# Attention with its last 64 keys as one product per pair of heads, and the first pair's prologue moved into the step lists

## What is computed

```python
# attention: B, H, S, D = 2, 8, 576, 64
scores = scale * np.matmul(q, k.transpose(0, 1, 3, 2))      # causal
a = exp(scores - max); a /= a.sum(-1) + 1e-9
local = np.matmul(a, v)
q_p = phi(q)                                                # max(q, 0) + min(exp(q), 1)
mem_out = (q_p @ M_prev) / (q_p . z_prev + 1e-6)
g = sigmoid(beta)
out = g * mem_out + (1 - g) * local
# then x = out as 1152 x 512: softplus(x @ w_in) @ w_out, and a mixture of 8 experts
```

## Time and profile before

| | |
|---|---|
| median of 3 runs | 1118.59 us (1118.3 to 1119.08) |
| the profiled execution | 1118.5 us, span 1116.5 us |
| granted TensorE clock, mean | 0.998 |
| PE busy | 1104.0 us (99%) |
| DVE, ACT, POOL busy | 703.5, 489.7, 434.4 us |
| attention (first to last pair's products) | up to about 147 us of the span |

### The profile page before, as it was taken

The page is one execution under the profiler, slowest core; times in us unless marked ns, Lnnn a source line. Parts: engine busy times, 40 slices in busy tenths (PEclk is TensorE's granted clock), DMA queues, the critical chain, the costliest instruction groups (busy, mean ns, idle before and its releaser), DMA issues.

```text
span 1116.5 us, 20453 instructions
## 1 busy us (share of the span) xinstructions
PE 1104.0 (99%) x6722; PEld 1004.2 (90%) x6722; DVE 703.5 (63%) x1319; ACT 489.7 (44%) x1061; POOL 434.4 (39%) x487
## 2 busy tenths in 40 slices
PE   7999999999999999999999999999999999999998
PEld 5889899999997989999899999999899899898997
DVE  5988743353377787666656666565675756657564
ACT  5888865575465333533333323333233332333331
POOL 5898800001044244253433534344352442524421
PEclk9999999999999999999999999999999999999999
DMA  4334122002001110101112011110111101111001
GB/s 110 90 98 108 32 76 75 1 1 77 0 20 38 38 47 30 57 23 54 57 38 56 19 56 56 38 56 19 56 56 38 56 19 56 53 39 41 19 10 76
DMA packets 65933, 52.78 MB, mean 47 GB/s; under 512 B 32480, under 2 KB 53984, under 8 KB 65888
## 3 DMA queue, kind: packets, MB, share of 16 engines
q1 hardware_dynamic: 65456, 52.13, 15.6%
q10 hardware_dynamic: 432, 0.07, 0.0%
HBM read 49.83 MB, written 2.36 MB: 47 GB/s over the span
## 4 chain that ended last, share of the span: by engine, by line
PE 94%; DVE 2%; issue 1%; POOL 1%; DMA 0%; ACT 0%; SPq 0%; ACTq 0%; POOLq 0%; DVEq 0%
PE ps_y L1474 40%; PE ps_h L1474 27%; PE ps_g L1474 17%; PE ps_o L1474 4%; PE ps_p L1512 2%; PE ps_s L1488 2%; PE ps_s L1474 0%; PE ps_y L1706 0%; DMA k_nat<-in_k_dram 0%; DVE zl L1235 0%; PE ps_t L1455 0%; PE ps_t L1459 0%; DVE acc L1355 0%; PE ps_g L1706 0%; PE ps_t L1466 0%
## 5 line engine op out<-in xcount | busy, mean ns | idle before, releaser
L898 ACT ACTIVATE zh<-h 128x256 fp32r<-128x256 f32 (+1 forms) x256 | 112.3, 444 | 329.3 <-POOL h L674 134.1
L1474 PE MATMUL ps_y<-w2c_h,zh 128*128 128x512 f32 x512 | 202.7, 396 | 0.0
L1474 PE MATMUL ps_y<-w2c_l,zh 128*128 128x512 f32 x512 | 201.8, 394 | 0.0
L1474 PE MATMUL ps_y<-w2c_h,zl 128*128 128x512 f32 x512 | 199.3, 389 | 0.0
L669 POOL TENSOR_TENSOR h<-u,p 128x256 f32<-128x256 f32 (+1 forms) x64 | 57.0, 891 | 361.9 <-DVE u L1212 361.9
L1235 DVE SCALAR_TENSOR_TENSOR zl<-h,zh 128x256 fp32r<-128x256 f32 (+1 forms) x256 | 173.1, 681 | 8.7 <-ACT zh L898 8.4
L1474 PEld LDWEIGHTS ps_y<-w2c_h,zl 128*128 128x128 f32 x512 | 96.2, 188 | 21.9
L1474 PEld LDWEIGHTS ps_y<-w2c_h,zh 128*128 128x128 f32 x512 | 96.6, 189 | 13.4
L1474 PEld LDWEIGHTS ps_y<-w2c_l,zh 128*128 128x128 f32 x512 | 96.6, 189 | 11.8
L1363 DVE SCALAR_TENSOR_TENSOR acc<-ps_y,weight,acc 128x512 f32<-128x512 f32 x112 | 82.2, 743 | 37.2 <-PE ps_y L1474 37.2
L674 POOL TENSOR_TENSOR h<-h,p 128x256 f32<-128x256 f32 (+1 forms) x64 | 60.9, 952 | 101.7 <-DVE h L1223 101.7
(11 more groups left out here) (243 smaller groups left out, 3056.2 us busy)
## 6 DMA issues: line engine op xcount, KB each, us to landing
rc<-in_moe_w_dram SPq DMA_DIRECT2D x64, 512.0 KB, 3.7
out_dram<-acc SPq DMA_DIRECT2D x9, 256.0 KB, 2.0
q_nat<-in_q_dram SPq DMA_DIRECT2D x16, 128.0 KB, 2.6
k_nat<-in_k_dram SPq DMA_DIRECT2D x16, 128.0 KB, 2.8
v_nat<-in_v_dram SPq DMA_DIRECT2D x16, 128.0 KB, 2.4
raw<-in_moe_w_in_dram SPq DMA_DIRECT2D x8, 256.0 KB, 3.0
raw<-in_moe_w_out_dram SPq DMA_DIRECT2D x8, 256.0 KB, 3.0
raw<-in_moe_w_in_dram SPq DMA_DIRECT2D x1, 2048.0 KB, 7.8
```

The costliest lines, as they stand in the source:

```text
L898: act.activation(z_place(u, quarter, 0), rows, ACT.Relu).then_inc(e_hi, 1)
L1474: last = pe.matmul(dst, a[x], b[y], start=start and i == 0, stop=stop and i == 2)
```

## The change

1. **One product for both heads' last keys.** The last 64 rows of v no longer go to `v_nat` (which keeps 4 blocks) but by one DMA per head into a second half of `mem_nat`, at the diagonal block of the head. `mem_h` and `mem_l` have two halves as well, split by the same two instructions, now of 256 columns; `vh` and `vl` shrink from 5 to 4 blocks. The transposed probabilities of the second head's tail go to partitions 64 to 127, which takes two instructions in place of one in `probs_hi` and `probs_lo` for the last part. `values(4, 1)` is then one product of full height: three matmuls of 256 columns in place of six of half height.
2. **The prologue as steps.** The straight code ahead of the lists is gone; its pieces stand in the first lists as `first`, `gate`, `relu0`, `phi0`, `keep0`, `split0`, `early`, in another order: GpSimd has `split0` 0 (`vh`, `mem_h`) ahead of `times_z`, `split0` 1 (`mem_l`) right after it, and `split0` 2 (`vl`) after `norm` 1; ScalarE has `relu` and `phi` ahead of `first` 2; VectorE has the norms ahead of `max` 2 and the row sums. The number of matmuls on zeros stays 22.
3. **Loads of the first pair.** q and k for both heads first (`ld_q0`, `ld_k0`), then both tails (`ld_t0`), then `z_prev` on SyncE's queue; `prep` 0 and 1 wait for the heads alone.
4. **New orders** in all eight lists. `split_v` has three parts, `keep` is a step of its own. In `PE_STEPS` "pt" 3 stands right behind "pt" 2, and "memory" 0 ahead of "prep" 3.

```diff
 PE_STEPS = [
-    ("qk", 5), ("pt", 2), ("qk", 6), ("pt", 3), ("prep", 3), ("memory", 0), ("pt", 4), ("pt", 5),
-    ("values", (0, 0)), ("values", (0, 1)), ("prep", 4), ("pt", 6), ("pt", 7),
+    ("qk", 5), ("pt", 2), ("pt", 3), ("qk", 6), ("memory", 0), ("prep", 3), ("pt", 4), ("pt", 5), ("values", (0, 0)),
+    ("values", (0, 1)), ("prep", 4), ("pt", 6), ("pt", 7),
 ]
 PE_FIRST = [
-    ("qk", 2), ("awake", 0), ("qk", 3), ("awake", 1), ("awake", 2), ("first", 3), ("awake", 3), ("qk", 4),
-    ("first", 4), ("prep", 0), ("pt", 0), ("pt", 1), ("prep", 1), ("awake", 4), ("awake", 5), ("memory", 0),
-    ("pt", 2), ("prep", 2), ("qk", 5), ("pt", 3), ("qk", 6), ("pt", 4), ("pt", 5), ("prep", 3), ("values", (0, 0)),
-    ("pt", 6), ("values", (0, 1)), ("prep", 4), ("pt", 7),
+    ("early", 0), ("early", 1), ("early", 2), ("early", 3), ("first", 0), ("first", 1), ("first", 2), ("qk", 0),
+    ("qk", 1), ("awake", 0), ("awake", 1), ("awake", 2), ("qk", 2), ("awake", 3), ("qk", 3), ("awake", 4),
+    ("first", 3), ("awake", 5), ("qk", 4), ("pt", 0), ("first", 4), ("prep", 0), ("pt", 1), ("pt", 2), ("memory", 0),
+    ("prep", 1), ("values", (0, 0)), ("pt", 3), ("prep", 2), ("pt", 4), ("qk", 5), ("qk", 6), ("values", (0, 1)),
+    ("prep", 3), ("pt", 5), ("pt", 6), ("prep", 4), ("pt", 7),
 ]
 DVE_STEPS = [
-    ("phi", 3), ("sum", 3), ("parts", 0), ("parts", 1), ("item", 2), ("sum", 4), ("x", -1), ("parts", 2),
+    ("parts", 0), ("phi", 3), ("parts", 1), ("sum", 3), ("x", -1), ("item", 2), ("max", 5), ("keep", 0), ("parts", 2),
...
 POOL_FIRST = [
+    ("split0", 0), ("phi0", 2), ("split0", 1), ("eps", 0), ("eps", 1), ("phi0", 4), ("norm", 0), ("norm", 1),
+    ("split0", 2), ("eps", 2), ("norm", 2), ("norm", 3), ("norm", 4), ("norm", 5), ("eps", 3), ("phi", 2),
+    ("norm", 6), ("split", 0), ("eps", 4), ("phi", 4), ("norm", 7), ("norm", 8), ("split", 1), ("eps", 5),
+    ("split", 2), ("weights", 0), ("norm", 9),
 ]
...
-            return to[1][0:TAIL, :, 4, 2 * P:2 * P + QB], bank[0:TAIL, 0:P].rearrange("p (h c) -> p h c", h=2)
+            rows = slice(h * QB, (h + 1) * QB)
+            return to[1][rows, 0, 4, 2 * P:2 * P + QB], bank[0:TAIL, rows]
...
+                if dst is v_nat:
+                    for h in range(2):
+                        sp.dma_start(mem_nat[h * QB:(h + 1) * QB, 1, h * D:(h + 1) * D],
+                                     both[h:h + 1, NT * P:S, :].rearrange("o p d -> p (o d)")).then_inc(done, 16)
+            def load_first():
+                for dst, src, done in ((q_nat, q3, ld_q0), (k_nat, k3, ld_k0)):
+                    for h in range(2):
+                        sp.dma_start(dst[:, 0:NT, h * D:(h + 1) * D],
+                                     src[h:h + 1, 0:NT * P, :].rearrange("o (j p) d -> p (o j) d", p=P))\
+                            .then_inc(done, 16)
+                for dst, src in ((q_nat, q3), (k_nat, k3)):
+                    sp.dma_start(dst[0:TAIL, NT, :].rearrange("p (h d) -> p h d", h=2),
+                                 src[0:2, NT * P:S, :].rearrange("h p d -> p h d")).then_inc(ld_t0, 16)
+                sp.dma_start(z_nat[:, 0, :], z3[:, 0:P].broadcast_to([P, P])).then_inc(ld_z[0], 16)
...
-                rows = slice(0, P if j < NT else TAIL)
-                for h in range(2):
-                    v_of = [x[rows, half, j, h:h + 2, :].rearrange("p a d -> p (a d)") for x in (vh, vl)]
-                    last = products(ps_o[:, c:n], v_of, [x[g][rows, h, j, c:n] for x in (pth, ptl)],
-                                    False, j == GKEYS[g] - 1 and h == 1)
+                if j < NT:
+                    for h in range(2):
+                        v_of = [x[:, half, j, h:h + 2, :].rearrange("p a d -> p (a d)") for x in (vh, vl)]
+                        last = products(ps_o[:, c:n], v_of, [x[g][:, h, j, c:n] for x in (pth, ptl)],
+                                        False, j == GKEYS[g] - 1 and h == 1)
+                else:
+                    last = products(ps_o[:, c:n], (mem_h[:, half, 1, :], mem_l[:, half, 1, :]),
+                                    [x[g][:, 0, j, c:n] for x in (pth, ptl)], False, True)
```

More of the change, by code:

```diff
@@ L37 @@
 ]
 ACT_FIRST = [
[L39 to L42, removed]
+    ("gate", 0), ("first", 0), ("first", 1), ("relu0", 0), ("phi0", 0), ("first", 2), ("exp", 0), ("exp", 1),
@@ L43 @@
+    ("exp", 2), ("exp", 3), ("exp", 4), ("exp", 5), ("first", 3), ("phi", 0), ("exp", 6), ("first", 4), ("parts", 0),
+    ("relu", 0), ("item", 0), ("exp", 7), ("parts", 1), ("parts", 2), ("item", 1), ("exp", 8), ("parts", 3),
+    ("item", 2), ("parts", 4), ("weights", 0), ("exp", 9), ("exp", 10), ("item", 3), ("parts", 5), ("x", 0),
+    ("parts", 6), ("item", 4),
 ]
@@ L55 @@
+    ("max", 2), ("keep0", 0), ("sum", 0), ("sum", 1), ("max", 3), ("first", 3), ("max", 4), ("first", 4),
+    ("parts", 0), ("sum", 2), ("phi", 1), ("item", 0), ("sum", 3), ("parts", 1), ("parts", 2), ("item", 1),
+    ("phi", 3), ("keep", 0), ("item", 2), ("max", 5), ("parts", 3), ("sum", 4), ("max", 6), ("parts", 4), ("item", 3),
+    ("parts", 5), ("sum", 5), ("x", 0), ("item", 4), ("parts", 6),
 ]
 POOL_STEPS = [
-    ("eps", 1), ("norm", 1), ("norm", 2), ("norm", 3), ("eps", 2), ("phi", 2), ("norm", 4), ("eps", 3), ("norm", 5),
@@ L624, in body @@
                         split_v(t, pair + 1, 1 - half)
-            times_z(0, 0)
-            eps(0, 0, 0)
-            pool.wait_ge(gates, 4)
-            scale_phi(0)
-            norm(0, 0, 0)
-            split_v(0, 0, 0)
-            split_v(1, 0, 0)
+                    elif what == "split0":
+                        split_v(t, 0, 0)
+                    elif what == "phi0":
+                        if t == 2:
+                            times_z(0, 0)
+                        else:
+                            scale_phi(0)
             pairs(pool, body)
@@ L1070, in phi @@
                     n = 4 * pair + 4
-                    if not isinstance(pair, int) or pair:
-                        dve.wait_ge(s_norm, 9 * pair)
-                    dve.tensor_tensor(keep[:, half:half + 1, :], keep_all[:, bass.ds(pair, 1), :],
-                                      ones[:, 0:3].unsqueeze(1), ALU.mult)
+                    if isinstance(pair, int) and pair == 0:
+                        dve.wait_ge(gates, 4)
                     dve.wait_ge(phi_z, pair + 2)
@@ L1108, in probs_lo @@
                 dve.wait_ge(p_hi, NB8 * pair + NB8 + b + 1)
-                to, bank = part_places(b, ptl)
-                less(to, bank, part_places(b, pth)[0]).then_inc(p_lo, 1)
+                for h in range(2 if b == NB8 - 1 else 1):
+                    to, bank = part_places(b, ptl, h)
+                    last = less(to, bank, part_places(b, pth, h)[0])
+                last.then_inc(p_lo, 1)
             def x_lo(g, pair, half):
@@ L1477, in scores @@
             def scores(t, pair, half):
+                if isinstance(pair, int) and pair == 0 and t == 0:
+                    pe.wait_ge(consts, 2)
                 pe.wait_ge(t_lo, 5 * pair + (8 if t == NS - 1 else 7))
@@ L1505, in probs @@
                 blocks, j0, j1 = PART[b]
+                if isinstance(pair, int) and pair == 0 and b == 0:
+                    pe.wait_ge(t_lo, 8)
                 pe.wait_ge(s_norm, 9 * pair + 9 + blocks[-1] + 1)
@@ L1516, in memory @@
             def memory(g, pair, half):
+                if isinstance(pair, int) and pair == 0 and g == 0:
+                    pe.wait_ge(zeroed, 1)
                 pe.wait_ge(o_lo, G * pair + g + G)
@@ L1521, in memory @@
                 c0, c1 = GCOLS[g]
-                products(ps_o[:, 0:c1 - c0], (mem_h[:, half, :], mem_l[:, half, :]),
+                products(ps_o[:, 0:c1 - c0], (mem_h[:, half, 0, :], mem_l[:, half, 0, :]),
                          [x[:, half, c0:c1] for x in (qph, qpl)], True, False)
```

175 lines of the change are left out of this document (96 added, 79 removed).

## The result

The changed kernel takes 1111.18 us (median of 4 runs, 1110.77 to 1111.79), against 1118.44 (4 runs, 1117.85 to 1119.08): a ratio of 0.9935, 95% interval 0.9918 to 0.9953. The forecast was 1112.7, its range 1110.4 to 1116.9. The profiled execution took 1110.8 us with a span of 1109.0, so 7.5 us of span are gone.

The account below looks back on a forecast made before the run. TensorE was taken as the bound, busy 1104.0 of 1116.5 us, with GpSimd's deliveries holding it in the first pair. 1118.5 - 3.2 (products) - 2.6 (prologue and loads), new orders at nothing, gave 1112.7 us; range 1110.4 to 1116.9.

Parts of the forecast that it names:

- Part 1: Attention's last-keys products on TensorE: three full-height matmuls for six half ones, 3.2 us saved over the eight pairs.
- the products save nothing: Rival on the last-keys products: half-height ones already overlap, so three full cost as much; 1115.9 us, chance 0.07.
- Part 2: First pair's prologue and loads: GpSimd's chain from `times_z` to `norm` 3 shortened, second pair's list earlier, 2.6 us saved.
- wait for the norms filled: GpSimd's prologue: the 1.80 us wait for the norms is filled with `mem_l` and two `eps`, about 0.7 us.
- the second issue then comes near 8.4 and lands near 11: M_prev load in the prologue: with `vh` and `mem_h` after it, `times_z` starts near 12.3, 0.6 us earlier.
- stays what it was: VectorE in the prologue: its work is unchanged, but it had idle time to give up, waiting for the norms.
- bound of 3.9: Upper bound of the prologue's gain: the wait for M_prev may vanish, some 1.3 us more than 2.6.
- Part 3: New orders of the engines' lists: costed at nothing.
- hazard: "pt" 3 right behind "pt" 2 on TensorE needs VectorE's later `ptl`; 0.2 to 0.5 us of cover, any excess paid seven times.
- waits of about 0.4 us per pair: Rival in the attention loop, from new orders or thinner cover: 1115.5 us, chance 0.10.
- the slower one: Rival: "pt" 3 waits for VectorE's `ptl` over 0.83 us per pair; at 1.2 us, 1121.1 us; chance 0.04.
- The clock may fall elsewhere, at the same price: TensorE's granted clock in the prologue, 0.50 in 24 to 26 us: a low stretch may move, its cost unchanged.

Follow-up runs that it names:

- the run with part 1 alone: Kernel before with only the full-height product for both heads' last keys, its loads and splits; old prologue and lists: 1115.17 us, ratio 0.9966.
- the run with `times_z` first: Changed kernel with GpSimd's `vh` and `mem_h` behind `times_z` in the first pair: 1110.92 us, ratio 0.993.
- the run with the old order of these loads and the old waits: Changed kernel with q's tail issued ahead of k and products waiting for heads and tail; `z_prev` stays on SyncE: 1110.9 us, ratio 0.9934.
- GpSimd's order alone: Kernel before with only GpSimd's prologue reordered: `vh` and `mem_h` ahead of `times_z`, `mem_l` right behind it: 1117.42 us, ratio 0.9992.
- The written-out kernel: Changed kernel with the loop over pairs 1 to 6 written out as straight code: 1110.37 us, ratio 0.9922.
- the run with part 1 undone: Changed kernel with six half-height products, v's tail and the splits as before; new lists stay: 1117.41 us, ratio 0.9987.
- the old lists: Changed kernel with its first pair's lists, but the old lists for all later pairs on all four engines: 1111.43 us, ratio 0.9939.
- both edits in the kernel before: Kernel before with the first pair's new loads and GpSimd's new prologue order; old lists and six half products stay: 1116.58 us, ratio 0.9983.
- the filled kernel: Kernel before with eight more matmuls on zeros in TensorE's first list, around `prep` 0 and the first "pt": 1118.16 us, ratio 0.9994.

## Why the prediction was right

Faster, and within the range: the forecast stood on two terms, the right ones. One was right by the run that isolates it; the other was mis-sized by 1.6 us, in part for causes that it did not have.

**Part 1 (3.2 us) was right**, and the run with part 1 alone is its clean test: 2.11 for six periods, where 1.9 was forecast, and 1.22 for the last stretch, where 1.27 was, together 3.33. In that run the last product to the first hidden one takes 0.12, as the prediction had it; TensorE's timeline:

```profile
144.65 0.28 PE L1485 MATMUL ps_o<-pth,mem_l 128*128 128x256 f32 x1
144.77 0.34 PE L1485 MATMUL ps_h<-xh,w1h 128*128 128x384 f32 x1
```

The changed kernel's 1.82 and 1.40 hold the new lists as well: they take back 0.3 of the 2.11, at the loop's end, and go with 0.18 more in the last stretch. That the ledger meets the forecast as closely as it does is partly luck. TensorE's timeline of the changed kernel has the three products of full height, 0.12 apart:

```profile
38.55 0.28 PE L1525 MATMUL ps_o<-pth,vl 128*128 128x256 f32 x1
38.67 0.28 PE L1525 MATMUL ps_o<-pth,mem_h 128*128 128x256 f32 x1
38.79 0.28 PE L1525 MATMUL ps_o<-ptl,mem_h 128*128 128x256 f32 x1
38.91 0.28 PE L1525 MATMUL ps_o<-pth,mem_l 128*128 128x256 f32 x1
39.12 0.39 PE L1541 MATMUL ps_s<-kh,qh 64*128 64x256 f32 x2
...
39.77 0.87 PE L1567 MATMUL ps_p<-ident,prob 128*128 128x128 f32 x6
```

From the last full product of v to the transposes are 39.77 - 38.55 = 1.22 us, where 1.25 was forecast and 1.57 stood before. That the products save nothing is dead: part 1 alone took 3.3 us or more off by itself. The rival stood on the up to 2x for a contraction of 64 or less in the Trainium skill's page "TensorEngine Tiling (Array Packing)", section "Theoretical Speedup", read as if it held for two products on the same rows; the trace doesn't bear that reading out. Half-height products that share their rows did not run side by side here.

**Part 2 (2.6 us) was right in mechanism and too small.** It gave 4.15 at norm 3, from these terms, by GpSimd's timelines of both profiles (in rounded numbers 4.16):

| term | forecast | measured |
|---|---|---|
| `times_z` starts earlier | 0.6 (at 12.3) | 1.69 (at 11.30) |
| `vh` and `mem_h` out of the stretch | 1.0 | 1.08 |
| wait for the norms filled | 0.7 | 0.42 (`mem_l`) + 0.38 (norms sooner) |
| `vl` shorter | 0.3 | 0.24 |
| norm 1 no longer slowed (0.63), less a new wait of 0.31 before norm 0 | 0 | 0.35 |
| sum | 2.6 | 4.16 |

The step that failed is "the second issue then comes near 8.4 and lands near 11". The M_prev issues began at 7.18, not 7.84 (I left out that v's issues took 1.64 before and 0.98 after), and landed 2.1 us after their issue, not 2.5: 10.0, and so `times_z` 1.0 us sooner than forecast. But the run with `times_z` first shows that its start alone is not what counts: 0.7 sooner still, it changed nothing, since GpSimd's own work then set `scale_phi`. Both paths begin with the loads. There the prediction named the wrong edit: it credited k's issue 0.74 earlier, and the run with the old order of these loads and the old waits lost nothing; the start of TensorE's transposes at 5.8 goes with `z_prev`. The sentence that VectorE's work "stays what it was" was the second miss: its order was worth 0.9 us in the profile. That `mem_l` can fill the wait for the norms hangs on the same reorder: with GpSimd's order alone it didn't. That the moved `z_prev` and VectorE's order came with the change was luck as far as the forecast goes; they made the gain larger than its bound of 3.9.

**Part 3 (0) was right as a sum, and its hazard was not the one.** "pt" 3 behind "pt" 2 cost nothing in any run; the idle time came where an iteration ends, 0.28 and 0.25 us, twice in all, and with six half products at "pt" 4. The written-out kernel, with every period at 15.02 or 15.03, took 0.85 us less for the six (0.8 by the medians). The rival "waits of about 0.4 us per pair" and the slower one did not happen; with six half products the first of them did (0.3 to 0.6 us per period over the kernel before). That the run with part 1 undone lost 6.2 us means that the terms of my sum, taken one at a time, hold only in one order of applying them: first the products, then the lists.

**The clock.** "The clock may fall elsewhere, at the same price" was half right: it fell nowhere in this profile, one of the four executions has a mean of 0.998, and in the profiles of other kernels it fell elsewhere. Norm 3 ended 4.15 us sooner, and in the kernel before it ended at 23.86, ahead of the stretch at 0.50 (22 to 24 had 0.84), so nearly all of the gain was there without the clock. From norm 3 to the second list are 10.50 us in the kernel before, with the low stretch, and 10.47 in the changed one, without it; but the work between them is in another order, so what the low stretch cost there can't be read off.

## What to carry to other kernels

In a kernel with one full engine, measure the distance between starts of the same instruction in consecutive iterations before and after, at the loop's end apart from the others: it separates a changed product, a changed order and a loop's cost to a twentieth of a microsecond. A product whose operands fill half the rows cost here as much as a full one, so packing two of them into one halved their cost; put the lists in order after it, since the order that was harmless with the short product lost 2.7 us with the long one. In a prologue, ask of each early load what lies ahead of it in any queue: here a transfer that nobody needed until 12.99 us went with a landing 1.2 us later of one that TensorE was waiting for.

## What the runs showed of the hardware

**A transfer from another queue.** `z_prev` (64 KB, to 128 partitions) issued from ScalarE's queue at 1.69 goes with a landing 1.2 us later of q's tail, issued from SyncE's at 1.81 (5.2 against 4.0 us; 5.8 with part 1 alone).

**The end of an iteration** went with 0.28 and 0.25 us of idle time on TensorE, and periods 0.31 to 0.34 us longer, with the new lists; with the old lists (15.12 and 15.11 inside, 15.17 and 15.14 across) with 0.03 to 0.06 us and no idle row, and written out with nothing (15.02 and 15.03 throughout).

**GpSimd beside VectorE.** Three of GpSimd's instructions took longer while VectorE ran an operation with two inputs in SBUF. `mem_h` of 128 columns took 0.30 us alone, and with both edits in the kernel before, GpSimd's and then VectorE's timeline:

```profile
10.94 0.86 POOL L593 TENSOR_SCALAR mem_h<-mem_nat 128x128 fp32r<-128x128 f32 x1
```

```profile
10.71 0.94 DVE L1091 SCALAR_TENSOR_TENSOR phi_e<-phi_e,phi_w 128x640 f32<-128x640 f32 x1
```

`vh` of the changed kernel takes 0.88 at 10.07 beside phi at 9.65, and 0.62 where it runs alone, at 12.11 in the run with `times_z` first. The Trainium skill, page "SBUF — State Buffer", section "SBUF: two separate sides", has the two engines share one pair of ports as a lock held for a whole instruction. The trace agrees for `mem_h`, which began 0.23 behind phi and ended at 11.80, 0.15 after phi. It doesn't agree for the others: norm 1 of the kernel before took 1.09 us at 21.69 beside phi at 21.71, against 0.46 for the same 128 columns at 17.85, though by these starts it was the first of the two; and `vh` lost only 0.26, less than a full wait for phi's end at 10.48 would be.

**The granted clock of a sparse prologue.** Low stretches stand in another place in each kernel's profile: 0.50 at 24 to 26 in the kernel before, at 16 to 20 in the filled one, at 10 to 12 in the written-out one, nowhere in the changed one. Between executions of one program only the mean is on record, and it differs too: 0.996 to 1.000 over the ten of the filled kernel, with 1120.01 and 1117.9 us at the ends.
